# Moving the early tokens' low parts ahead of two query tiles, and two weight splits into the first expert step

## What is computed

```python
def phi(x):                                   # attention features, FEAT = 128
    proj = einsum('bhsd,df->bhsf', x, w_phi)
    proj = proj - max(abs(proj), axis=-1)
    return concatenate([exp(proj), exp(-proj)], axis=-1)
q_p, k_p = phi(q), phi(k)
kv, z = einsum('bhsf,bhsd->bhfd', k_p, v), sum(k_p, axis=2)
attn = einsum('bhsf,bhfd->bhsd', q_p, kv) / (einsum('bhsf,bhf->bhs', q_p, z) + 1e-6)

x = attn.transpose(0, 2, 1, 3).reshape(2304, 512)      # mixture of 8 experts
e_idx = argmax(x @ w_gate)
for e in range(8):
    h = relu(x[e_idx == e] @ w1[e])                     # 512 -> 1024
    out[e_idx == e] = gate_w * sigmoid(x @ w_output_gate)[e] * (h @ w2[e])

xn = x / sqrt(mean(x * x) + 1e-6) * rms_g               # FFN of width 1536
y = (silu(xn @ w_gate) * (xn @ w_val)) @ w_out
```

## Time and profile before

| | us |
|---|---|
| median of the runs | 909.52 |
| lowest and highest of the 3 runs | 904.52, 909.9 |
| the profiled execution, its own time | 900.01 |
| its span, first to last instruction | 898.3 |
| TensorE busy | 875.0 (97%) |
| VectorE, ScalarE, GpSimd busy | 430.7, 294.0, 123.0 |
| mean granted TensorE clock | 0.994 of full |

### The profile page before, as it was taken

How to read it: one execution, slowest core, us unless ns; L and a number is a source line. 1 busy time by engine, 2 the same in 40 slices (tenths; PEclk the granted TensorE clock), 3 DMA queues, 4 the chain that set the end, 5 groups by cost and what they waited for, 6 DMA issues and landing times.

```text
span 898.3 us, 16710 instructions
## 1 busy us (share of the span) xinstructions
PE 875.0 (97%) x6432; PEld 794.5 (88%) x6433; DVE 430.7 (48%) x875; ACT 294.0 (33%) x479; POOL 123.0 (14%) x145
## 2 busy tenths in 40 slices
PE   8999999999999999999899999999999999999996
PEld 6776859588999999999899999999999999999996
DVE  5688888997587434443456422222222222222222
ACT  4555545652356333222444321121121112112111
POOL 1010203033234221125200010010000001001001
PEclk9999999999999999999999999999999999999998
DMA  8614614021754444328633720030020002000000
GB/s 280 201 54 176 225 53 158 2 81 40 256 149 119 80 79 65 69 30 183 153 128 119 178 88 1 1 106 1 1 70 35 0 25 80 0 0 36 1 1 36
DMA packets 37185, 75.37 MB, mean 84 GB/s; under 512 B 8176, under 2 KB 24688, under 8 KB 35472
## 3 DMA queue, kind: packets, MB, share of 16 engines
q1 hardware_dynamic: 32832, 56.07, 23.5%
q0 software_dynamic: 3488, 17.85, 5.4%
q10 hardware_dynamic: 816, 0.79, 0.3%
HBM read 51.06 MB, written 23.64 MB: 83 GB/s over the span
## 4 chain that ended last, share of the span: by engine, by line
PE 85%; DVE 8%; issue 3%; ACT 2%; DMA 1%; POOL 0%; DVEq 0%; POOLq 0%; SPq 0%; ACTq 0%
PE ps L1025 11%; PE ps L1027 10%; PE ps L1026 10%; PE ps L1040 5%; PE ps L1041 5%; PE ps L1039 5%; PE ps L927 4%; PE ps L928 4%; PE ps L929 4%; PE ps L940 3%; PE ps L942 3%; PE ps L941 3%; PE ps L768 3%; PE ps L823 2%; PE ps L728 2%
## 5 line engine op out<-in xcount | busy, mean ns | idle before, releaser
L1025 PE MATMUL ps<-xnH,blkH 128*128 128x384 f32 x576 | 194.6, 338 | 3.3 <-DVE blkL L1692 2.3
L1027 PE MATMUL ps<-xnH,blkL 128*128 128x384 f32 x576 | 194.2, 337 | 0.0
L1026 PE MATMUL ps<-xnL,blkH 128*128 128x384 f32 x576 | 194.1, 337 | 0.0
L1699 DVE TENSOR_TENSOR sg<-sg,ps 128x384 f32<-128x384 f32 x72 | 39.9, 554 | 246.6 <-ACT sg L1258 246.6
L1258 ACT ACTIVATE sg<-ps 128x384 f32<-128x384 f32 x72 | 35.4, 491 | 253.2 <-PE ps L1027 253.2
L1025 PEld LDWEIGHTS ps<-xnH,blkH 128*128 128x128 f32 x576 | 108.8, 189 | 7.5 <-issue 4.7
L1026 PEld LDWEIGHTS ps<-xnL,blkH 128*128 128x128 f32 x576 | 108.9, 189 | 2.7
L1027 PEld LDWEIGHTS ps<-xnH,blkL 128*128 128x128 f32 x576 | 108.8, 189 | 0.0
L1040 PE MATMUL ps<-blkL,hH 128*128 128x512 f32 x216 | 84.9, 393 | 0.0
L1041 PE MATMUL ps<-blkH,hL 128*128 128x512 f32 x216 | 84.8, 393 | 0.0
L1039 PE MATMUL ps<-blkH,hH 128*128 128x512 f32 x216 | 84.6, 391 | 0.0
(11 more groups left out here) (219 smaller groups left out, 1552.5 us busy)
## 6 DMA issues: line engine op xcount, KB each, us to landing
stage<-in_ffn_w SPq DMA_DIRECT2D x12, 768.0 KB, 4.3
xin<-xs_dram SPq DMA_DIRECT2D x9, 578.2 KB, 9.9
xs_dram<-zrow SPq DMA_DIRECT2D x8, 578.2 KB, 8.0
qT<-in_q SPq DMA_DIRECT2D x4, 1152.0 KB, 6.5
xnH_dram<-xoH SPq DMA_DIRECT2D x8, 576.0 KB, 3.5
xnL_dram<-xoL SPq DMA_DIRECT2D x8, 576.0 KB, 4.9
xnH<-xnH_dram SPq DMA_DIRECT2D x6, 768.0 KB, 4.9
xnL<-xnL_dram SPq DMA_DIRECT2D x6, 768.0 KB, 6.3
```

The lines of the kernel that those rows point to most:

```text
L1025: e.matmul(o, hi, xnH[par][:, c, :], start=(c == 0), stop=False)
L1026: e.matmul(o, hi, xnL[par][:, c, :], start=False, stop=False)
L1027: last = e.matmul(o, lo, xnH[par][:, c, :], start=False, stop=(c == KC - 1))
```

## The change

```diff
-        split_slots_dve = [(B - 1, sl) for sl in (1, 2, 5, 6, 7, 8, 9)] + [(B, 0)]
+        split_slots_dve = [(B - 1, sl) for sl in (1, 2, 5, 6, 7, 8)]
...
@@ tensor, step(par, g, begin) @@
+                    if m == 6 and begin > 0:
+                        e.wait_ge(s["sp_lo"], PIECES)
                     if m > 1:
                         outputs(par, g, m - 2)
...
@@ tensor, the tail @@
             slot(B, 1)
             with e.If(early > 0):
                 e.wait_ge(s["dve_XT"], KC)
-                once(0, 0)
+                e.wait_ge(s["sp_hi"], PIECES)
+                e.wait_ge(s["sp_lo"], PIECES - 2)
                 hidden(0, 0, 0)
...
@@ vector, the tail @@
-            slot(B, 1)
             with e.If(early > 0):
                 take_rows(0, XT_FIRST)
                 for name in ("dve_ms", "dve_R", "dve_xn", "dve_xl"):
                     e.sem_inc(s[name], 1)
+            slot(B, 1)
             slot(B, 2)
             slot(B, 3)
             early_low(0)
             slot(B, 4)
             early_low(1)
             early_low(2)
+            split_low(PIECES - 2, 0, PIECES - 1)
             route_3(B)
...
             link(e.tensor_tensor(key, key, active, ALU.add))
             early_low(3)
+            split_low(PIECES - 1, 0, PIECES)
```

## The result

| | before | changed |
|---|---|---|
| median of 20 runs each, us | 906.16 | 910.62 |
| lowest and highest | 902.63, 909.9 | 905.57, 913.3 |
| profiled execution, its span | 898.3 | 908.9 |

The ratio is 1.0046 with a 95% interval of 1.0032 to 1.0061: the change costs 2.9 to 5.5 us. I had forecast 910.4 us and within 1%, and both hold, but that the time came out at 910.62 is luck. The base that I added to, 909.52, was the median of three runs; that of 20 runs is 906.16, which is 3.4 us lower. And the cost that I added, 0.9 us, is too small by a factor of four to five (4.5 us between the medians, 4.2 by the ratio). The two errors cancel. The question of this study is where the rest of the cost comes from.

The account below looks back on a forecast made before the run. TensorE was taken to bound the kernel, with VectorE setting the pace almost as much in the changed stretch. -1.5 + 2.28 - 0.24 + about 0.35 = +0.9 us, added to 909.52, gave 910.4 us; range 902.5 to 912.5.

Parts of the forecast that it names:

- the two splits: On VectorE behind `early_low(2)` and `early_low(3)`: 1.14 us each, 2.28 us in front of `early_low(4)`.
- the exclusion of VectorE and GpSimd: Second split beside the scatter: if the rule held for scatters, the sum would be about 1.3 us higher; costed at nothing.
- `xmL` ahead of tile (3, 8): VectorE makes the four `xmL` earlier; TensorE's first wait shrinks from 1.96 to 0.5 us and `hidden(2)` starts 1.5 us earlier.
- slack: Between the end of `early_low(4)` and the start of `hidden(6)` in the old profile: 0.24 us, subtracted from the cost.
- restart: From the end of `early_low(4)` to TensorE's start of `hidden(6)`: 0.14 to 0.47 us, entered as about 0.35.
- causes that the trace doesn't show: Explanation for the median of runs shown lying 9.5 us above the profiled execution; taken as untouched by the change.
- becomes idle time: Attention's tail on VectorE: most of the 2.87 us of splits taken out turns into waiting for the first `xmH`.
- The half clock in the new stall: Rival: TensorE's clock halves after the 1.9 us idle in front of `hidden(6)`; +2.5 us in all, 912.0; chance 0.35.
- The gain survives: Rival: unseen air in VectorE's chains hides both splits, so the 1.5 us gain stays; 908.0 us; chance 0.10.
- nothing happens to the first wait: Rival: reading `early` or the branch lies open in front of `xmL`, so -1.5 is missing; at least 911.9; chance 0.05.
- The chances by 1%: Whole kernel's time: faster by over 1% 0.02, within 1% 0.96, slower by over 1% 0.02.

Follow-up runs that it names:

- e1: The kernel before, unchanged, timed and profiled a second time; ratio 0.9991, median 903.99 us.
- e3: The kernel before with only the four `xmL` moved ahead of tile (3, 8), splits left in place; ratio 1.0006 to the kernel before.
- e7: The kernel before with one redundant split of piece 7 added in slot (B, 0), making VectorE late; ratio 1.0024 to the kernel before.
- e2: The changed kernel, unchanged, timed and profiled a second time; ratio 1.0037 to the kernel before.
- e8: The changed kernel with one redundant split of piece 6 added in slot (B, 0); ratio 1.0038 to the kernel before.

## Why the prediction was right and wrong

**The changed kernel's own stretch: right, nearly to the tenth.** On the scale of positions I had forecast `hidden(0)` at 2.94, `hidden(2)` at 7.3 to 7.7, and `hidden(6)` at 23.1 to 23.4. The first comes at 2.52, the others at 7.67 and 23.07. VectorE's idle time in front of `xmL` was forecast as 2.6 and is 2.50, TensorE's in front of `hidden(6)` as 1.9 and is 1.70; the stall in front of `hidden(5)`, forecast as 0.25 to 0.55, is 0.14. That `hidden(0)` is 0.4 us early is the part of the change that I had missed: I carried over the 0.47 us between the last `xmL` and `hidden(0)`, of which 0.4 went with `once`. It changes nothing further on, since VectorE holds `hidden(2)` back. From `early_low(2)` to `early_low(4)` VectorE took 235.57 - 226.94 = 8.63 us in e1 and 240.04 - 229.13 = 10.91 in the changed kernel: 2.28 more, exactly the two splits at 1.14. The split beside the scatter took 1.22, so the exclusion of VectorE and GpSimd that the Trainium skill states ("SBUF — State Buffer", "SBUF: two separate sides") cost VectorE nothing there. I looked at the split alone, though. The scatter beside it is the one that got longer:

```profile
234.38 0.97 POOL L613 DMA_INDIRECT xs_dram<-x5s,pos  x1 [0.30 <-issue]
235.66 1.66 POOL L613 DMA_INDIRECT xs_dram<-x5s,pos  x1 [0.30 <-issue]
```

The split ran from 235.27. The 20 scatter instructions of this profile have a median of 0.96 us, and the one other long one, 1.62 at 199.82, also has a split beside it (199.45 to 200.67). Of the pair in the earlier trace rows the scatter took 1.33. So the two do get in each other's way, and it is GpSimd that pays, for which TensorE never waits in this stretch. Beside a GpSimd copy VectorE paid again, with 1.65 in e1 at 214.64.

**The step that failed: "`xmL` ahead of tile (3, 8)", -1.5 us.** I measured it against a `hidden(2)` at 215.51, position 9.20. In the usual execution the old kernel has it at 6.71. Of the 2.5 us between the two, 1.0 was VectorE's late position and the rest TensorE's half clock, both passing states of that one execution. I call e1 the usual one because e3 and e7, whose lists on VectorE are the same up to there, have the split ahead of tile (3, 7) at -4.48 and -4.41, as e1 has (211.83 - 216.31 = -4.48), and not at 202.83 - 206.31 = -3.48. Against the usual position `hidden(0)` gains 0.9 (0.5 from `xmL`, as in e3, and 0.4 from `once`), and `hidden(2)` *loses* 0.96, as e3 shows alone. `early_low(2)` then starts at 11.65 instead of 10.63. So the sum should have been +1.02 + 2.28 - 0.24 (slack) + 0.05 (restart) = +3.1, which e1 and e2 show, instead of -1.5 + 2.28 - 0.24 + 0.35 = +0.9. The restart, too, was mis-sized: `hidden(6)` starts 0.05 us after `early_low(4)` ends (240.55 against 240.04 + 0.46). The 3.1 lies inside the intervals of both timings (2.9 to 5.5 and 1.8 to 4.9 us).

**What I should have weighed.** The prediction notes that the profiled execution, 900.01 us, lay 9.5 below the median, and puts that down to "causes that the trace doesn't show". It lay 4.5 us below the lowest of the three runs shown, too. That was the sign that this execution was not one to take a base of waits from. What it lacked was the pauses of TensorE in the numerators, of which the nine later profiles show 3.9 to 5.6 us each. These pauses delay TensorE against VectorE. That they are the reason why VectorE is usually 1.0 us better placed in the tail fits the ten profiles, but I didn't switch them off, so it is argued, not shown. What e7 and e8 show is that VectorE's position in the tail alone changes what the edit is worth, by 1.2 us.

**What I had called free.** I wrote that most of the 2.87 us taken out of VectorE's list "becomes idle time" and costed the delay of tiles (3, 8) and (3, 9) at nothing, since VectorE idled 1.34 us in front of `early_low(0)`. In the usual execution that cover is gone: `early_low(0)` follows at once (222.12 in e1, no idle time in front). Of the idle time of 2.5 us that the change makes in front of `xmL`, the last 1.0 is paid for there, from -0.1, when tile (3, 8) could have started, to 0.91. In e3 VectorE idles for only that long, and `hidden(2)` comes at the same 7.67.

**The rivals.** The half clock in the new stall (0.35) didn't come. Neither of the changed kernel's two profiles has it behind its stalls of 1.68 and 1.70, or 1.69 and 1.67 us, and over all timed runs with which the second was taken the mean granted clock is 0.9955 for the changed kernel (12 runs) and 0.9953 for the one before (35 runs). "The gain survives" and "nothing happens to the first wait" fell as well. The chances by 1% held: a cost of 0.4% is within 1%.

## What to carry to other kernels

Before a sum of tenths of a us is built on the waits of one profile, compare that execution's time with the runs: if it lies outside them, a second profile of the unchanged kernel is worth more than all further reading. Moving an engine's work "ahead" of other work is only free if the engine isn't made to wait there while the work it could do stands behind; here half a us gained on the first matmuls cost a whole one two chunks later. And work that is moved off a busy list must go where the list is idle: the same two splits cost 2.1 us behind `early_low(2)` and `early_low(3)`, and nothing ahead of `early_low(2)` and behind `early_low(5)`. And what an edit drops by the way is part of it: 0.4 us went with a helper whose waits alone I had counted.

## What the hardware showed that I had not expected

- A dense stream of narrow matmuls (64x81, one every 38 ns) has pauses of 0.2 to 1.1 us that nothing releases, at about the same three slots of attention in nine of ten profiles, 3.9 to 5.6 us in all, and none in the tenth. They are followed by half clock in some cases (at 202.5 in the changed kernel's first profile, behind pauses of 0.84, 0.41 and 0.40) and not in others (nowhere in e7 and e8). What causes them stays open.
- The length of an idle time alone does not decide whether the clock halves. 1.96 us was followed by half clock in the old profile, 2.21 us in the same place of e7 was not. What else differed between the two executions stays open.
- Most of the spread between runs goes with the granted clock. Of the changed kernel's 20 runs, the three with a mean clock of 0.991 took 912.8 to 913.3 us, the two with 0.998 and 0.999 took 905.6 and 906.1.
- After VectorE's release TensorE's next matmul started 240.55 - 240.50 = 0.05 us later in the changed kernel's profile, less than the 0.14 to 0.47 that I had as bounds. The 0.47 contained the increments in `once`.
